# Three edits to a chained kernel on one core: scatter placement in attention, the shape of the expert loop, and the order of the first dense products

## The reference

```python
# attention: B, H, S, D = 4, 8, 768, 48
for t in range(S):
    cur = einsum('bhd,bhe->bhde', u * k[t], v[t])
    y[t] = einsum('bhd,bhde->bhe', r[t], state + cur)
    state = w * state + einsum('bhd,bhe->bhde', k[t], v[t])
x = y as 3072 tokens of 384

# experts: E = 8, F = 1024; only tokens with x @ w_skip > 0, each to its best expert
out = x; e = argmax(x @ w_gate); gain = softmax(x @ w_gate)[e]
out[chosen] = x + gain * (relu(x @ w1[e]) @ w2[e])

# dense: F = 2048
h = out @ w_in
result = (h * clip(h + 3, 0, 6) / 6) @ w_out
```

## Time and profile before

| what | us |
| --- | --- |
| median of 3 runs | 712.52 (711.06 to 712.73) |
| the profiled execution | 712.61 |
| its span, first to last instruction | 710.8 |
| PE busy | 699.3 |
| DVE, ACT, POOL busy | 385.6, 320.9, 139.4 |
| mean granted clock of PE | 0.998 of full speed |

### The profile page before, as it was taken

How to read it: one execution, slowest core, us unless ns; L and a number is a source line. 1 busy time by engine, 2 the same in 40 slices (tenths; PEclk the granted TensorE clock), 3 DMA queues, 4 the chain that set the end, 5 groups by cost and what they waited for, 6 DMA issues and landing times.

```text
span 710.8 us, 13909 instructions
## 1 busy us (share of the span) xinstructions
PE 699.3 (98%) x5202; PEld 636.6 (90%) x5202; DVE 385.6 (54%) x803; ACT 320.9 (45%) x699; POOL 139.4 (20%) x190
## 2 busy tenths in 40 slices
PE   7999999989999999999999999999999999999998
PEld 5888888889999999889999999999999999998997
DVE  6677668777888888665534334333333343334332
ACT  4777667715555555554433333333333333323222
POOL 8747866541232222100000000000000000000000
PEclk9999999999999999999999999999999999999999
DMA  9688876717666667400011002000200020001001
GB/s 187 132 192 189 189 159 157 232 33 253 229 222 236 213 211 247 128 31 1 0 51 40 0 1 89 1 0 1 90 0 1 1 90 0 1 1 45 1 1 44
DMA packets 106762, 65.71 MB, mean 92 GB/s; under 512 B 79764, under 2 KB 102296, under 8 KB 106704
## 3 DMA queue, kind: packets, MB, share of 16 engines
q1 hardware_dynamic: 102896, 60.31, 29.7%
q0 software_dynamic: 2560, 4.60, 2.0%
q10 hardware_dynamic: 1248, 0.02, 0.1%
HBM read 53.37 MB, written 12.48 MB: 93 GB/s over the span
## 4 chain that ended last, share of the span: by engine, by line
PE 95%; ACT 2%; issue 1%; DVE 1%; DMA 1%; DVEq 0%; POOL 0%; SPq 0%; ACTq 0%; POOLq 0%
PE bank_A L965 8%; PE bank_A L966 8%; PE bank_A L964 8%; PE bank_L L964 4%; PE bank_L L966 4%; PE bank_L L965 4%; PE bank_P L965 4%; PE bank_P L964 4%; PE bank_P L966 4%; PE bank_kT L965 4%; PE bank_kT L966 4%; PE bank_kT L964 3%; PE bank_A L881 3%; PE bank_YT L966 3%; PE bank_YT L965 3%; PE bank_YT L964 3%
## 5 line engine op out<-in xcount | busy, mean ns | idle before, releaser
L1436 DVE TENSOR_TENSOR g_lo<-g,g_hi 128x512 fp32r<-128x512 f32 x96 | 66.4, 692 | 67.0 <-ACT g_hi L757 67.0
L757 ACT ACTIVATE g_hi<-g 128x512 fp32r<-128x512 f32 x96 | 60.7, 632 | 73.1 <-DVE g L1434 73.1
L1434 DVE SCALAR_TENSOR_TENSOR g<-cut,bank_A 128x512 f32<-128x512 f32 x60 | 41.2, 687 | 92.9 <-ACT cut L754 92.9
L754 ACT ACTIVATE cut<-bank_A 128x512 f32<-128x512 f32 x60 | 35.9, 598 | 101.4 <-PE bank_A L966 100.8
L966 PE MATMUL bank_A<-mT_hi,wi_lo 128*128 128x512 f32 x180 | 71.0, 394 | 0.0
L965 PE MATMUL bank_A<-mT_lo,wi_hi 128*128 128x512 f32 x180 | 70.9, 394 | 0.0
L628 ACT ACTIVATE bank_A<-ident,own 128x128 f32<-128x128 f32 x188 | 58.2, 356 | 26.7 <-DVE A_sb L1167 21.0
L964 PE MATMUL bank_A<-mT_hi,wi_hi 128*128 128x512 f32 x180 | 70.0, 389 | 0.0
L1434 DVE SCALAR_TENSOR_TENSOR g<-cut,bank_kT 128x512 f32<-128x512 f32 x36 | 24.7, 687 | 66.7 <-ACT cut L754 66.7
L754 ACT ACTIVATE cut<-bank_kT 128x512 f32<-128x512 f32 x36 | 21.5, 598 | 70.1 <-PE bank_kT L966 70.1
L964 PE MATMUL bank_kT<-mT_hi,wi_hi 128*128 128x512 f32 x108 | 42.1, 389 | 0.9 <-DVE mT_lo L1427 0.9
(11 more groups left out here) (271 smaller groups left out, 1858.9 us busy)
## 6 DMA issues: line engine op xcount, KB each, us to landing
raw<-in_moe_w_dram SPq DMA_DIRECT2D x24, 512.0 KB
raw<-in_moe_w_dram SPq DMA_DIRECT2D x7, 1536.0 KB
r_in<-in_r_dram SPq DMA_DIRECT2D x24, 192.0 KB, 3.6
k_in<-in_k_dram SPq DMA_DIRECT2D x24, 192.0 KB, 3.8
v_in<-in_v_dram SPq DMA_DIRECT2D x24, 192.0 KB, 3.5
x_scratch<-y_sb SPq DMA_DIRECT2D x24, 192.0 KB, 2.2
m_in<-x_scratch SPq DMA_DIRECT2D x5, 768.0 KB, 5.1
out_dram<-o_sb SPq DMA_DIRECT2D x10, 384.0 KB, 2.7
```

The source lines that it names most:

```text
L754: eng.activation(cut[f % 2][:, :], p_H[f % 3][:, :], ACT.Relu, bias=0.5, scale=1.0 / 6.0).then_inc(s_cut, 1)
L757: eng.activation(g_hi[f % 4][:, :], g[f % 2][:, :], ACT.Copy).then_inc(s_ghi, 1)
L1434: eng.scalar_tensor_tensor(g[f % 2][:, :], cut[f % 2][:, :], 1.0, p_H[f % 3][:, :], ALU.min, ALU.mult).then_inc(s_g, 1)
L1436: eng.tensor_tensor(g_lo[f % 4][:, :], g[f % 2][:, :], g_hi[f % 4][:, :].bitcast(F32), ALU.subtract).then_inc(s_glo, 1)
```

## The change

Three edits. In attention, from chunk 2 on, POOL issues one indirect transfer after each of the four steps of a chunk, where it issued two after the first and two after the second. The expert loop becomes pair 0, a loop over the pairs 1 to 3 and, if there are more than 8 tiles, a second loop over the pairs 4 to 10; the test inside `pair` stays. PE's first piece of the first dense block takes the six matmuls with `mT_hi` of all three parts first, each part behind a wait for its `s_mhi`, and then the three with `mT_lo`, behind `s_mlo`; it had taken the three matmuls of each part together.

```diff
--- before.py
+++ after.py
@@ -31,8 +31,8 @@
 SPARE = TH * P - TT
 MAXT = (N + E * (TT - 1)) // TT
 MAXT += MAXT % 2
-ROUNDS = 2
-PAIRS = -(-(MAXT // 2 - 1) // ROUNDS)
+PAIRS = MAXT // 2
+FIRST_PAIRS = E // 2
 NK = -(-N // TT)
 NK += -NK % (P // math.gcd(TT, P))
 EC = NK * TH
@@ -311,10 +311,11 @@
         def expert_loop(eng, n_tiles, pair):
 
             pair(0, 0)
-            with eng.Fori(0, ROUNDS) as group:
-                with eng.If(n_tiles > group * (2 * PAIRS) + 2):
-                    with eng.Fori(group * PAIRS + 1, group * PAIRS + PAIRS + 1) as m:
-                        pair(m * 2, m)
+            with eng.Fori(1, FIRST_PAIRS) as m:
+                pair(m * 2, m)
+            with eng.If(n_tiles > 2 * FIRST_PAIRS):
+                with eng.Fori(FIRST_PAIRS, PAIRS) as m:
+                    pair(m * 2, m)
 
         def dense_loop(eng, block_step):
 
@@ -527,8 +528,7 @@
             for c in range(2, NC):
                 for b in range(B):
                     step(b, c)
-                    if b in (0, 1):
-                        scatters(c - 2, c - 2, range(b * 2, b * 2 + 2))
+                    scatters(c - 2, c - 2, range(b, b + 1))
                 identify(c)
             scatters(NC - 2, NC - 2, range(B))
             def fetch(i):
@@ -1081,9 +1081,17 @@
                     eng.wait_ge(s_g, G2 * blk + (f - 1 if f < 2 else f - 2) + SHIFT)
                     if first:
                         eng.wait_ge(s_wilo, f + 1)
+                    if first and f == 0:
+                        for kc in range(KC):
+                            eng.wait_ge(s_mhi, kc + 1)
+                            eng.matmul(p_H[0][:, :], wi_hi[:, kc, 0:P], mT_hi[i][:, kc, :], start=kc == 0, stop=False)
+                            eng.matmul(p_H[0][:, :], wi_lo[:, kc, 0:P], mT_hi[i][:, kc, :], start=False, stop=False)
+                        for kc in range(KC):
+                            eng.wait_ge(s_mlo, kc + 1)
+                            a = eng.matmul(p_H[0][:, :], wi_hi[:, kc, 0:P], mT_lo[i][:, kc, :], start=False, stop=kc == KC - 1)
+                        a.then_inc(s_H, 1)
+                        continue
                     for kc in range(KC):
-                        if first and f == 0:
-                            eng.wait_ge(s_mlo, kc + 1)
                         piece = slice(f * P, (f + 1) * P)
                         a = three(p_H[f % 3][:, :], wi_hi[:, kc, piece], wi_lo[:, kc, piece],
                                   mT_hi[i][:, kc, :], mT_lo[i][:, kc, :], kc == 0, kc == KC - 1)
```

## The result

| | before | after |
| --- | --- | --- |
| median, us | 712.52 | 716.01 (715.79 to 716.73, 5 runs) |
| ratio, 95% interval | | 1.0056 (1.0040 to 1.0072) |
| span of the profiled execution, us | 710.8 | 714.2 |

The changed kernel is 3.5 us slower than before, which is outside the forecast's range of 710.6 to 714.2. Two stretches lose, and the profile of after shows both.

The account below looks back on a forecast made before the run. PE, busy 699.3 of 710.8 us, was taken to bound the kernel. Attention 0 and the hand-over -0.33 us (302.06 against 302.39), from a median of 712.52, gave 712.2 us; range 710.6 to 714.2.

Parts of the forecast that it names:

- Cost on the path: 0: Attention: one scatter per step moves waits lying beside PE work, so costs PE nothing; bounds -1.5 to +1.2 us.
- theory A: Attention, follow-up forecast: DVE's carry copy is held 2.6 us during POOL's unbroken row; 0.7 to 2.5 us slower.
- a jump to a page that PE had not fetched: Expert exit: dense code moves about three pages on, so PE's jump finds unfetched code; 1.3 us taken for the fetch.
- PE's code comes ahead of its use: PE's instruction queue: PE keeps more code than it is running and fetches one page ahead.
- 0.5 + 1.3: Expert exit on PE: 0.5 us for loop end and test with jump, plus 1.3 us for fetching code.
- I take the middle, 298.1: Expert exit: PE's instruction stream arrives at 298.1 us, between its last wait (297.18) and last product (298.97).
- 0.5 + 2.5: Expert exit on PE, upper bound: 0.5 us of turns plus 2.5 us for a load ahead of the packet and the packet.
- 0.27 us a turn: Expert exit: each loop turn or jump costs 0.27 us, read from ACT's 1.60 us of issue over six.
- 299.9: Hand-over to dense: PE's instruction stream goes on at 299.9 us, after turns and fetch; bounds 297.7 to 302.0.
- rival (b): Expert exit: a 3 us fetch on every engine, PE resuming at 301.6, ACT's gains late; +2.3 us, 714.8; chance 0.12.
- At best 0.7 us: First dense piece: six high-part products start before mT_lo is ready, so the next piece comes up to 0.7 us earlier.
- 0 and -0.33: Total: 0 us for spreading scatters in attention, -0.33 us for loop and high parts first at the hand-over.

Follow-up runs that it names:

- e10: Kernel before with the new expert loop (pairs 1 to 3, test, second loop) in PE's program only, old loop on the other four engines; ratio 1.0043.
- e11: Kernel before with the new expert loop on the other four engines, PE keeping the old loop; ratio 1.0005.
- e4: Kernel before with expert loop groups of three and seven pairs sharing one body, dense code staying next to it; ratio 1.0006.
- e9_fill: Changed kernel with 18 identity transposes on PE behind the last expert products and ahead of the jump; ratio 1.0103.
- f3: Kernel before with groups of three and seven pairs sharing one body, high-part matmuls first, and a one-element reduce for DVE's carry; ratio 0.9966.
- f5: Kernel before with groups of three and seven pairs sharing one body and high-part matmuls first, carry still a copy; ratio 0.9981.
- e2_loop: Kernel before with only the new expert loop (pairs 1 to 3, test, second loop), on all engines; ratio 1.0039.
- e5_carry: Changed kernel with DVE's carry done as an addition of zero in place of the copy; ratio 1.0090.

## Why the prediction was wrong

**Edit 1.** The step "Cost on the path: 0", with bounds of -1.5 and +1.2 us, is wrong: 2.6 us, beyond both. What it reasoned holds: the waits of own for `ruk` were not on PE's path, and those of PE at b=0 were DVE's routing chain. But a change to POOL's order was priced only by semaphores, by who waits for what POOL writes. DVE and POOL meet in another way, which the trace of before showed: the carry took 0.16 us in chunk 1 and 0.5 to 0.8 in the four in which POOL was at work. That row was not read; its group costs under 3 us in all. The size of the hold could not be read from it, since there it ended with one product of POOL. The upper bound should have allowed for the whole row that POOL does without a break, after the change scatter, iota, `k_dec` and `rk`, about 3 us, in a chain that the prediction itself had found to bound PE.

The runs tell three forms apart, at the same moment of POOL's row: 2.58 us for the copy, 2.57 for the addition, 0.16 for the reduce. The length differs with the place: in the kernel before, the hold ended with one instruction of POOL; in the long cases it outlasted a scatter, an iota and two products. What it is that DVE waits for there no run shows: the "port" of theory A was the author's guess at a cause, and what is shown is the forms and the times.

**Edit 2.** The mechanism, a jump to a page that PE had not fetched, was right and is borne out by `e10`, `e11` and `e4` (ratios of 1.0043, 1.0005 and 1.0006) and by the new packets on q8. A page in the prediction is such a packet of 16 KB (16 of 0.26 MB in the earlier trace rows). That q8 brings PE's code was taken there from the number of instructions alone; `e10` and `e11` show it, with two packets between 293 and 301 us when the new loop is PE's and none when it is the others'. That PE's code comes ahead of its use was inferred from rows, and two things that were measured agree with it. PE worked 405.50 of the 408.40 us from 302.40 on the earlier trace rows, with 16 packets from 300 on the earlier trace rows, so they cannot each have held it for the 1.0 us that the one at 312 took. And in all five profiles with the new loop in PE's program (`e9_fill` among them) one packet starts 0.9 to 1.0 us before the gap and the next only 0.3 to 0.5 us after PE's first dense product, with no idle of PE of 0.4 us or more behind that until 312 us: in the changed kernel they start at 299.1 and 302.5, around 299.65 and 302.01, in `e10_far_pe` at 297.4 and 300.7, around 297.90 and 300.32. How far ahead PE's code is brought in general, and how much of it PE keeps beyond the 2.5 pages of a pair's body, the runs do not show.

The term that was mis-sized is "0.5 + 1.3", turns and fetch. From PE's last product to the first dense one it is 2.4 to 2.7 us in four profiles, so more than 1.8 even if PE's stream comes to the exit only with that product. It came somewhat earlier: an exit like the old one took ACT 1.60 us and held PE for 1.25 behind its last product, and one like that of `f3` took ACT 0.74 and held PE for at most 0.25, which gives an estimate of 0.4 to 0.5 us ahead, if turns cost PE what they cost ACT. So "I take the middle, 298.1" was early by some 0.4 us, and turns and fetch together took about 2.8 to 3.1, at the upper bound of 0.5 + 2.5. How the two share it is open; ACT's 0.1 us shows that 0.27 us a turn does not hold for every exit. PE resumed at 302.01 in a trace that runs 0.68 us later there (299.65 against 298.97), so at 301.3 on the clock of before, inside the bounds of 297.7 to 302.0 but far from 299.9.

**The clock.** It was in no term. The prediction let PE resume at full speed after any gap, in the forecast and in rival (b). With PE's gap of 0.9 us it is at 1.00 in the earlier trace rows; that a fall costs 1.7 us of PE's work stood in the same trace, at 148 us. Of rival (b)'s +2.3 us for the hand-over the size came near the 2.7 of the trace. Its part on PE, resuming at 301.6, was nearly right (301.3); its part on ACT was not: the others' exits cost nothing (`e11`), ACT's shrank to 0.1 us. The clock stood in its place, which is luck. How much of the time hangs on the clock is itself not settled: the one execution of after with a mean clock of 1.000 took 716.56 us, no less than the others.

**Edit 3.** "At best 0.7 us" stands as a bound, and the sum that gave it nearly nothing behind a late exit was right; `f5` and `f3` reach it once the exit is short (3.11 us to the next piece becomes 2.42).

**The sum.** By the runs with one edit each: +2.6, +2.8 and -0.8 us, 4.6 in all, against 4.0 for the three together (0.56%), which the intervals cover. Of the 2.8 the profiles show 1.1 to 1.4 as PE's later start and 1.7 as its clock, where that fell; but a fall also comes elsewhere and in the kernel before, so that the second part holds on average and not in each execution. The forecast had 0 and -0.33.

## What to carry to other kernels

When POOL's order changes, price it against every instruction of DVE beside it, not only against its waiters: look for a small instruction whose longest duration is several times its shortest (here 0.78 and 0.16 us in the kernel before), and ask what happens if it falls into the longest unbroken row (here 2.58 us). A loop body that was written twice, so that the run skipped the second, put a jump into unfetched code in front of what follows, 2.8 us here (`e2_loop`); one body with bounds that depend on the group has as short an exit without it (`e4_groups`, 1.0006). A gap on PE costs itself and perhaps the clock behind it: a clock of 0.50 for some 3.5 us, 1.7 us of PE's work, behind three of the five gaps of 2 us at the hand-over. And since the clock fell in the kernel before as well (at 148 us), compare the mean clocks of the executions before a difference of 1 or 2 us is put down to an edit.

## What the runs showed of the hardware that was not expected

A copy (or an addition) of 8 numbers a partition on DVE was held for 2.55 to 2.58 us in twelve places of six kernels, always through scatter, iota and two products of POOL; these came 0.55 to 0.58 us into a scatter. Where one came 0.0 to 0.25 us into a scatter it was not held at all (0.16 to 0.20 us), and where one fell into a product it was held until about that product's end (0.27 to 0.87 us). PE's jump to unfetched code took 2.4 to 2.7 us from its last product, the same jump on ACT 0.1 us. Fillers ahead of the jump did not hide it: 18 of 2.13 us in all moved the next product by 2.2 us. And of five gaps of PE between 1.98 and 2.29 us at the hand-over, three (the changed kernel, `e2_loop`, `e5_carry`) were followed by a clock of 0.50 and two (`e10_far_pe`, `e9_fill`) were not; behind the shorter gaps there it stayed up. At the turn from attention to the experts PE waited 1.9 to 2.3 us for the first tile's rows in 17 of the 20 profiles, and the clock fell to 0.50 behind 11 of these waits; in the other three it fell ahead of that wait, in the kernel before with no idle of PE over 0.47 us.
